# Where the second network's rounding runs, when the first network's last sums leave their banks, and when the last weights are split

## The reference

```python
h = np.maximum(x @ w_in, 0.0)            # first network, 1536 tokens, 512 -> 2048
x = h * h @ w_out                        # 2048 -> 512

h = x @ w_in2                            # second network, same sizes
P = a[0] + a[1] * h + a[2] * h**2 + a[3] * h**3
Q = 1.0 + np.abs(b[0]) * np.abs(h) + np.abs(b[1]) * h**2
out = (P / (Q + 1e-06)) @ w_out2
```

## Time and profile before

| | |
|---|---|
| median of 3 runs | 607.12 us (606.97 to 607.15) |
| profiled execution, device time | 609.34 us |
| profiled execution, span from first to last instruction | 607.6 us |
| PE, PEld | 590.7 us (97%), 481.3 us (79%) |
| DVE, ACT, POOL | 444.5 us (73%), 263.7 us (43%), 153.6 us (25%) |
| mean granted TensorE clock | 0.994 |

### The profile page before, as it was taken

One profiled execution on the slowest core, in us unless ns is written; L12 is line 12 of the kernel. 1 busy time (PEld: TensorE's weight loads), 2 busy tenths in 40 slices (PEclk: granted clock), 3 DMA queues, 4 the chain that ended last, 5 costly groups with the idle time before them and its releaser, 6 DMA issues.

```text
span 607.6 us, 10584 instructions
## 1 busy us (share of the span) xinstructions
PE 590.7 (97%) x3770; PEld 481.3 (79%) x3770; DVE 444.5 (73%) x834; ACT 263.7 (43%) x564; POOL 153.6 (25%) x163
## 2 busy tenths in 40 slices
PE   7988999999999999999999899999999999999996
PEld 4877788888888888888888677788888888888884
DVE  5878796664433323466674799999999999999996
ACT  4988611011310111301112855556766665766554
POOL 3679810000300000400000755521222212222220
PEclk9999999999999999999999999999999999999998
DMA  8883470000000000022232000000100000100001
GB/s 260 256 236 116 150 277 0 1 0 1 1 0 0 0 0 0 35 81 93 105 105 104 35 1 0 1 0 1 69 0 0 0 0 0 71 0 1 0 1 69
DMA packets 11186, 31.42 MB, mean 52 GB/s; under 512 B 1552, under 2 KB 2064, under 8 KB 11152
## 3 DMA queue, kind: packets, MB, share of 16 engines
q1 hardware_dynamic: 10864, 30.68, 15.3%
q10 hardware_dynamic: 288, 0.26, 0.1%
HBM read 27.79 MB, written 3.15 MB: 51 GB/s over the span
## 4 chain that ended last, share of the span: by engine, by line
PE 49%; DVE 35%; issue 8%; ACT 4%; POOL 3%; DVEq 1%; POOLq 0%
PE bank L520 22%; PE bank L587 21%; DVE ratio L982 9%; DVE numer L964 6%; DVE ratio L976 5%; DVE numer L962 5%; DVE ratio L971 5%; DVE hhi L989 4%; ACT prob L668 2%; POOL prob L354 1%; PE bank L602 1%; PE bank L506 1%; PE bank L490 1%; POOL vwin L339 1%; PE bank L545 1%
## 5 line engine op out<-in xcount | busy, mean ns | idle before, releaser
L520 PE MATMUL bank<-xhi,whi 128*128 (+1 forms) x384 | 149.9, 390 | 0.0
L520 PE MATMUL bank<-xhi,wlo 128*128 (+1 forms) x384 | 149.4, 389 | 0.0
L520 PE MATMUL bank<-xlo,whi 128*128 (+1 forms) x384 | 149.4, 389 | 0.0
L407 POOL TENSOR_TENSOR denom<-denom,habs 128x512 f32<-128x512 f32 (+1 forms) x49 | 62.2, 1271 | 252.5 <-ACT denom L746 252.5
L685 ACT ACTIVATE hsq<-bank 128x512 f32<-128x512 f32 x48 | 28.8, 600 | 213.2 <-PE bank L520 213.1
L520 PEld LDWEIGHTS bank<-xhi,wlo 128*128 128x128 f32 x384 | 72.2, 188 | 15.2
L520 PEld LDWEIGHTS bank<-xhi,whi 128*128 128x128 f32 x384 | 72.2, 188 | 15.0
L520 PEld LDWEIGHTS bank<-xlo,whi 128*128 128x128 f32 x384 | 72.0, 188 | 14.7
L602 PE MATMUL bank<-whi,hhi 128*128 128x512 f32 x192 | 76.8, 400 | 6.2 <-DVE hlo L993 6.2
L602 PE MATMUL bank<-wlo,hhi 128*128 128x512 f32 x192 | 76.2, 397 | 0.0
L602 PE MATMUL bank<-whi,hlo 128*128 128x512 f32 x192 | 75.9, 396 | 0.0
(11 more groups left out here) (76 smaller groups left out, 896.3 us busy)
## 6 DMA issues: line engine op xcount, KB each, us to landing
wraw<-w SPq DMA_DIRECT2D x32, 512.0 KB, 3.3
vwin<-vw SPq DMA_DIRECT2D x16, 288.0 KB, 5.2
out<-osb SPq DMA_DIRECT2D x12, 256.0 KB, 2.1
kraw<-kT SPq DMA_DIRECT2D x7, 384.0 KB, 5.3
q<-qT SPq DMA_DIRECT2D x7, 384.0 KB, 4.1
kraw<-kT SPq DMA_DIRECT2D x2, 128.0 KB, 2.3
q<-qT SPq DMA_DIRECT2D x1, 256.0 KB, 4.9
kraw<-kT ACTq DMA_DIRECT2D x1, 128.0 KB, 2.8
```

The lines of the kernel that those rows point to most:

```text
L407: g.tensor_tensor(denom[:, i, cols], denom[:, i, cols], habs[:, i, cols], ALU.mult).then_inc(q_done, 1)
L520: last = mm(hps[j % 2][:, :], W[a][:, j, kt * P:(kt + 1) * P], X[b][:, kt, bass.ds(CH * c, CH)], start=kt == 0 and i == 0, stop=kt == KT - ...
```

## The change

1. The rounding of `ratio` to `hhi` (`high`) moves from VectorE to ScalarE. On ScalarE the rounding of tile m-1 stands inside `terms` of tile m, behind its `denom` and ahead of its `numer`. For the last tile, which is done in two halves, the roundings stand behind both exponentials. VectorE's order for the two halves of the last tile is changed with it.
2. The four banks of the first network's last sums are emptied by four plain copies (`y_raw`) that stand behind tile 1's reciprocal, where eight copies stood between tile 1's `terms` and its reciprocal. Each bank's rounded copy (`y_hi`) is made later from `xraw`, one behind each of the tiles 2 to 5. GpSimd takes the four differences behind the tiles 13, 15, 17 and 19. The row copies of a finished chunk (`rows_out`) also move behind tile 1's reciprocal.
3. `LATE` is 3 and not 4, so VectorE splits the weights of tile 12. GpSimd splits the six halves of the tiles 13 to 15 behind the tiles 0, 3, 5, 7, 9 and 11, the halves for `hidden` first, where it split eight halves behind the tiles 2 to 9. The sums of the tiles 13 to 15 wait for their own half (`late_out`).

The core of the diff:

```diff
-LATE = 4
+LATE = 3
...
-        product(0, 0)
-        product(1, 1)
-        y_lo(NCH - 1)
-
-        for x in range(2 * LATE):
-            product(2 + x, x % 2)
-            j = FT - LATE + x // 2
+        def split_late(j, half):
             index, turn = landing(FT + j)
             pool.wait_ge(w_in[index], 16 * (turn + 1))
-            split(half_slot(j, x % 2), w_hi_pool, 2 * EARLY + x, w_late)
...
+        product(0, 0)
+        split_late(FT - 3, 0)
+        product(1, 1)
+        between = [None, lambda: split_late(FT - 2, 0), lambda: split_late(FT - 1, 0)]
+        between += [lambda j=j: split_late(j, 1) for j in range(FT - LATE, FT)]
+        between += [lambda dt=dt: y_lo_last(dt) for dt in range(KT)]
+        for pair in range(1, len(between)):
+            product(2 * pair, 0)
+            product(2 * pair + 1, 1)
+            between[pair]()
...
+            if j >= FT - LATE:
+                pe.wait_ge(late_out, j - FT + LATE + 1)
...
-                        pe.wait_ge(ylo_done, KT * NCH)
+                        pe.wait_ge(ylo_done, KT * c + 2 * KT)
...
+        def y_raw(dt):
+            bank_done(y_done, NCH - 1, dt, KT, STEPS - 1)
+            a.copy(xraw[last_y(dt)], acc[dt][:, :].unsqueeze(1)).then_inc(y_free, 1)
+
+        def y_hi(dt):
+            act.wait_ge(y_free, done(KT, KT * (NCH - 1) + dt))
+            a.copy(xhi[last_y(dt)], xraw[last_y(dt)]).then_inc(yhi_done, 1)
...
+        def high(m, i, cols=WHOLE, tile=None):
+
+            act.wait_ge(ratio_done, m + 1)
+            act.wait_ge(b_done, done(2, STEPS + (m if tile is None else tile) - 2))
+            a.copy(hhi[:, i, cols], ratio[:, cols]).then_inc(hi_done, 1)
...
-            for cols in parts:
+            for part, cols in enumerate(parts):
                 a.activation(denom[:, i, cols], habs[:, i, cols], ACT.Identity, bias=cb[:, 0:1],
                              scale=cb[:, 1:2]).then_inc(den_done, 1)
+                if part == 0 and not first:
+                    high(m - 1, 1 - i)
...
+        rational(0, 0, first=True)
+        rational(1, 1)
+        for dt in range(KT):
+            y_raw(dt)
+        for dt in range(KT):
+            rational(2 + dt, dt % 2)
+            y_hi(dt)
...
+        for half, cols in enumerate(HALVES):
+            high(LAST + half, 1, cols, LAST)
         rows_out(NCH - 1)
...
-            for step in (newton_1, newton_2, product, high, low):
+            for step in (newton_1, newton_2, product, low):
                 step(m, i, i)
...
         newton_1(*first)
         newton_2(*first)
+        product(*first, LAST)
         newton_1(*second)
-        product(*first, LAST)
         newton_2(*second)
-        high(*first, LAST)
+        low(*first)
         product(*second, LAST)
-        low(*first)
-        high(*second, LAST)
         low(*second)
```

More of the change, by code:

```diff
@@ L212, in build @@
     w_in_ready, w_out_hi, w_out_ready = sem("w_in_ready"), sem("w_out_hi"), sem("w_out_ready")
-    w_late = sem("w_late")
+    late_in, late_out = sem("late_in"), sem("late_out")
     h_full = sem("h_full")
@@ L393, in _, with y_lo @@
             split_out(j)
-        def y_lo(c):
+        def y_lo(c, dt):
+            part = (slice(None), dt, slice(CH * c, CH * (c + 1)))
+            g.tensor_tensor(xlo[part], xraw[part], xhi[part].bitcast(F32), ALU.subtract).then_inc(ylo_done, 1)
+        for c in range(NCH - 1):
             for dt in range(KT):
                 pool.wait_ge(y_free, done(KT, KT * c + dt))
[L398 to L402, removed]
+                y_lo(c, dt)
         def product(m, i, cols=WHOLE):
@@ L407, in product, with y_lo_last @@
             g.tensor_tensor(denom[:, i, cols], denom[:, i, cols], habs[:, i, cols], ALU.mult).then_inc(q_done, 1)
-        product(0, 0)
-        product(1, 1)
-        y_lo(NCH - 1)
-        for x in range(2 * LATE):
-            product(2 + x, x % 2)
-            j = FT - LATE + x // 2
+        def split_late(j, half):
             index, turn = landing(FT + j)
             pool.wait_ge(w_in[index], 16 * (turn + 1))
-            split(half_slot(j, x % 2), w_hi_pool, 2 * EARLY + x, w_late)
-        with pool.Fori(2 + 2 * LATE, STEPS - 2, 2) as m:
+            split(half_slot(j, half), w_hi_pool, 2 * EARLY + LATE * half + j - FT + LATE, (late_in, late_out)[half])
+        def y_lo_last(dt):
+            pool.wait_ge(yhi_done, KT * (NCH - 1) + dt + 1)
+            y_lo(NCH - 1, dt)
+        product(0, 0)
[8 more added lines that the diff above has]
+            between[pair]()
+        with pool.Fori(2 * len(between), STEPS - 2, 2) as m:
             for i in range(2):
@@ L528, in weights_ready @@
             elif index >= 2 * FT - LATE:
-                pe.wait_ge(w_late, 2 * (index - 2 * FT + LATE + 1))
+                pe.wait_ge(late_in, index - 2 * FT + LATE + 1)
             else:
@@ L723, in y_out, with last_y @@
                 a.copy(xraw[part], acc[dt][:, :].unsqueeze(1)).then_inc(y_free, 1)
+        def last_y(dt):
+            return slice(None), slice(dt, dt + 1), slice(CH * (NCH - 1), TOK)
+        def y_raw(dt):
[4 more added lines that the diff above has]
+            a.copy(xhi[last_y(dt)], xraw[last_y(dt)]).then_inc(yhi_done, 1)
         relu(1, 1)
@@ L735, in _, with terms @@
                     relu(FT * c + j + i, i)
-        def terms(m, i, parts=(WHOLE,)):
+        def high(m, i, cols=WHOLE, tile=None):
+            act.wait_ge(ratio_done, m + 1)
+            act.wait_ge(b_done, done(2, STEPS + (m if tile is None else tile) - 2))
+            a.copy(hhi[:, i, cols], ratio[:, cols]).then_inc(hi_done, 1)
+        def terms(m, i, parts=(WHOLE,), first=False):
             n = STEPS + m
@@ L756, in reciprocal, with rational @@
             a.activation(rcp0[bank][:, cols], rcp0[bank][:, cols], ACT.Exp, scale=-1.0).then_inc(r0_done, 1)
[L758 to L761, removed]
+        def rational(m, i, first=False):
+            terms(m, i, first=first)
             reciprocal(m, i, i)
@@ L770, in _, with tiles, chunk @@
         act.wait_ge(coef_step, 3)
[L771 to L774, removed]
+        def tiles(c, first, last):
+            with act.Fori(first, last, 2) as j:
                 for i in range(2):
                     rational(FT * c + j + i, i)
-        chunk(0, lambda: y_out(NCH - 1))
+        def chunk(c, last=FT):
+            rational(FT * c, 0)
+            rational(FT * c + 1, 1)
+            rows_out(c - 1)
+            tiles(c, 2, last)
+        rational(0, 0, first=True)
[5 more added lines that the diff above has]
+            y_hi(dt)
+        tiles(0, 2 + KT, FT)
         with act.Fori(1, NCH - 1) as c:
-            chunk(c, lambda: rows_out(c - 1))
-        chunk(NCH - 1, lambda: rows_out(NCH - 2), final=True)
+            chunk(c)
+        chunk(NCH - 1, FT - 2)
         rational(LAST - 1, 0)
@@ L983, in product @@
                                    ALU.subtract, ALU.mult).then_inc(ratio_done, 1)
[L985 to L989, removed]
         def low(m, i, bank, cols=WHOLE):
```

## The result

The changed kernel takes 599.73 us in the median of 6 executions (598.44 to 602.83), the kernel before on the same chips 608.12 us (6 executions, 606.97 to 610.51). The ratio is 0.9872, with a 95% interval of 0.9849 to 0.9895: 1.3% faster, some 7.8 us; the two medians lie 8.39 apart. The prediction had 598.7 us and a range of 597.2 to 602.0.

The account below looks back on a forecast made before the run. It took TensorE, busy 97% of the span, plus its waits for `hlo` as the bound. Gains of 8.12 us at the change of networks and 0.3 at the end, 8.4, off 607.12 gave 598.7 us, range 597.2 to 602.

Parts of the forecast that it names:

- The change of networks: From the second network's sums 0 to sums 9: waiting 2.28, slow clock 1.74, slow tiles 4.10, all recovered, 8.12 us.
- The layout of one tile: Steady tile, from its `habs` start: `hlo` done at 8.8 us, sums want it at 10.7, 1.9 us to spare.
- The margins of the race: `ratio` starts ahead of GpSimd's next product by 0.7 us in steady tiles, 0.2 at tiles 2, 18 and 34.
- the 4.10 us of the slow stretch: Seven steps, sums 2 to 9, where VectorE and GpSimd block each other: 4.10 us lost, put at fully recovered.
- The end: Last two sums: gaps of 0.5 and 1.7 us, last matmul 1.4 us earlier, less 1.1 for clock, gain 0.3.
- the clock: Gap ahead of sums 47 may halve TensorE's clock, costing 2.2 us; half of it, 1.1, taken off the gain.
- the sum: 8.12 us at the change of networks plus 0.3 at the end: 8.4 us off 607.12, giving 598.7.
- Rival 1: GpSimd's product starts before `ratio`: 5.9 us a tile; 611.1 us from tile 18, 618 from tile 2; chance 0.10.
- Rival 2: `ratio` starts late from tile 2, won back by tile 8 or so: costs about 4 us, 602.8 us; chance 0.06.

Follow-up runs that it names:

- e4: The changed kernel with the weight halves as before (LATE 4, eight halves behind tiles 2 to 9): 601.94 us, ratio 0.9897.
- e8: The changed kernel with the rounding to `hhi` back on VectorE: 606.25 us, ratio 0.9966.
- e3: The kernel before with only the weight halves moved (LATE 3, VectorE splits tile 12): 606.11 us, ratio 0.9970.
- e2: The kernel before with only the bank and row copies and GpSimd's four differences moved, rounding on VectorE: 607.25 us, ratio 0.9992.
- e12: The changed kernel with bank copies, row copies and GpSimd's four differences where they were before: 626.11 us, ratio 1.0267.
- e1: The kernel before with only the rounding to `hhi` moved to ScalarE: 626.79 us, ratio 1.0268.
- e6: The changed kernel with an unused 256-column copy added on ScalarE behind the row copies of chunks 1 and 2: 614.86 us, ratio 1.0117.
- e9: The changed kernel run again, unchanged, in six more executions: 599.61 us, ratio 0.9841.
- e11: The changed kernel with each group's fourth copy behind `denom` of the chunk's tile 2, plus an unused 256-column ScalarE copy: 601.58 us, ratio 0.9889.
- e5: The changed kernel plus an unused 64-column ScalarE copy behind chunks 1 and 2's row copies: 598.64, 599.12, 612.95 and 614.36 us; ratio 0.9846 for the short two.
- e10: The changed kernel with each group's fourth copy behind tile 2's `denom`, and tile 46's rounding behind both halves of tile 47's `denom`: 601.16 us, ratio 0.9878.

## Why the prediction was right

**The change of networks, 8.12 us.** All of it came back: the steps 0 to 11 lose nothing. The layout of one tile held: in tile 10 `hlo` is done 8.80 us behind that tile's `habs`, where the prediction has 8.8, and the sums start at 10.60, where it has 10.7. The rounding takes 0.62 us where 0.66 was put in, as the group of ACT shows; with it the groups of DVE and POOL, 320 to 600 us (busy us, mean ns, idle before):

```profile
L1029 DVE TENSOR_TENSOR hlo<-ratio,hhi 128x512 fp32r<-128x512 f32 x47 | 50.1, 1065 | 34.6 <-ACT hhi L764 34.6
L1024 DVE SCALAR_TENSOR_TENSOR ratio<-numer,ca,ratio 128x512 f32<-128x512 f32 x47 | 35.3, 752 | 5.7
L764 ACT CAST hhi<-ratio 128x512 fp32r<-128x512 f32 x47 | 29.1, 620 | 13.1 <-DVE ratio L1024 12.2
L407 POOL TENSOR_TENSOR denom<-denom,habs 128x512 f32<-128x512 f32 x47 | 64.3, 1368 | 241.5 <-ACT denom L775 241.5
```

`ratio` takes 0.75 us in every tile; in a steady tile before it was 1.28. `hlo` is lengthened instead, to 1.07 in the mean, where TensorE has slack, and VectorE idles 34.6 us for the rounding at no cost. (The Trainium skill, VectorE: DVE Perf Modes, the cycle table under the TRN2 errata, gives an estimate of 0.61 us for this rounding; the trace agrees, 0.62.)

The margins of the race were forecast as 0.2 at tile 2, 0.2 at tiles 18 and 34 and 0.7 in between. The trace has 0.11, 0.19 and 0.20, and 0.71 in the steady stretch. After each of the three the margin comes back by 0.1 a tile. The timeline of DVE and POOL after, at tile 2:

```profile
345.86 0.75 DVE L1024 SCALAR_TENSOR_TENSOR ratio<-numer,ca,ratio 128x512 f32<-128x512 f32 x1
...
345.97 1.79 POOL L407 TENSOR_TENSOR denom<-denom,habs 128x512 f32<-128x512 f32 x1 [3.55 <-ACT denom L775]
```

**What it did not see.** The prediction took the 4.10 us of the slow stretch as recovered by all parts together, with the rarer weight halves named as one reason. The runs put it down to the rounding: without the halves' new places it is all recovered (e4), without the rounding only 0.3 of it is (e8, 3.8 lost). The halves alone gave 2.6 us (e3, of which 2.2 in the first two steps). And the four differences on GpSimd, which the prediction passed over, would cost 1.9 us in the steps 12 to 19 if VectorE still rounded (e2, e8). What the rounding hides is thus 3.8 + 1.9 + 0.2 at these places and 1.4 at the end (there together with VectorE's new order for the last tile, which e8 also takes back): 7.3 of the 9.49. The copies and the splits give the other 2.2, and the copies keep the race from being lost at tile 1 (e12).

**The end.** The gaps were to be 0.5 and 1.7 us. Counted as the prediction counts them, by how much later the sums start than they could, they are 0.49 and 1.78; the idle times in the rows are 0.33 and 1.53. The last matmul was to start 10.1 behind the last tile's `habs`, and it starts 10.12 behind it (583.81 to 593.93). The loss at the end is 2.4 instead of 3.8, the 1.4 of the prediction. The term that was off is the clock: the prediction took off 1.1, half of what a lower clock would cost in the last sums, and the profiled execution shows none, nor does any other with a gap of 1.48 to 1.53 us at this place (e1, e4, e6, e9, e11). This is the difference between the 9.49 measured and the 8.4 of the sum. That the median lies 1.0 above the forecast all the same is not explained by a step of it: the kernel before has a median of 608.12 over six executions and of 607.12 over the three from which the forecast subtracted. So it is luck in part that the two medians lie 8.39 apart and the sum has 8.4: the sum contains a clock cost of 1.1 that no trace of this kernel shows.

The end also shows that the low clock before was not what made it late. In e8 (and e2) the gap ahead of sums 46 is as long, the clock stays at 1.00, and the end loses the same 3.8 us, because a second gap opens ahead of sums 47. The slow matmuls before had only covered that wait. What came back is the shorter way to the last `hlo`. PE in e8, and the window behind the first gap:

```profile
593.45 0.47 PE L613 MATMUL bank<-whi,hhi 128*128 128x512 f32 x1 [1.95 <-DVE hlo L1031]
...
597.73 0.47 PE L613 MATMUL bank<-whi,hhi 128*128 128x512 f32 x1 [1.31 <-DVE hlo L1031]
...
593.40:597.70 4.30, 2.97 (x12) 2.17 (x12) 4.23 (x11) 0.00 (x0) 0.00 (x0) 1.00 0.00 0
```

**Rival 1** is real, and its price was right. It was worked out as 5.9 us a tile and is 5.80 to 5.87, with `ratio` at 1.46 us and not near 1.2. From tile 18 it was to cost 12.4 us; the e5 execution that lost there loses 15.7 from sums 0 on against 2.4, so 13.3, and took 612.95 against the 611.1 of the prediction. The prediction let a start be decided by 0.1 us and gave this case 0.10. In 12 executions of the changed kernel it did not come true: the highest is 602.83, and where the race was lost at tile 18 the time was above 612. Lost at tile 34 it would cost, as an estimate from the same rows, 12 tiles of 0.4 us and the 1.8 by which the end of e5 is dearer, some 6.6.

**Rival 2**, a loss won back, was not seen in a trace. Once lost, the margin does not grow back: in e12 it is -0.38 us in nearly every tile from 12 to 45. In e5 it was won once, at tile 33, where the row copies push GpSimd's next product 2.0 us back (tile 34's `habs` comes 7.86 us behind tile 33's, where 5.8 is usual in this state), and lost again in the next tile.

**What stays open.** Of the 12 executions of the changed kernel (e9's with it) three lie at 601.89 to 602.83 us, with a mean granted clock of 0.997 or 0.994; the nine at 598.4 to 600.9 have 1.000. None of the three was profiled. A race lost for good it is not, since that costs 6.6 us at the least. The profiled execution of e4 (601.29 us, mean clock 0.997) shows one place where such time can lie: from sums 0 on it loses 2.3 us like the changed kernel, but far ahead of the networks, in the attention, its clock is lowered. The windows from 30 to 45 us, of e4 and then of the changed kernel:

```profile
30.00:45.00 15.00, 13.04 (x302) 10.38 (x296) 10.50 (x59) 10.95 (x49) 9.19 (x13) 0.89 0.69 216
...
30.00:45.00 15.00, 13.77 (x368) 11.06 (x360) 12.26 (x71) 13.14 (x59) 11.17 (x16) 1.00 0.83 241
```

The profiled execution of e6, the longest of its four, has 0.77 from 15 to 30 us and 0.89 from 30 to 45, and its sums 0 start at 345.18. Nor does a wide margin make the scatter smaller (e10: 600.09 to 603.72, e11: 600.67 to 605.17). The short loss at tile 2 that rival 2 describes is thus not needed to explain these executions, but no run rules it out. Whether the 0.11 us at tile 2 is always enough is open too: 0.08 was in two traces, 0.05 was not in one.

## What to carry to other kernels

Where two engines share a resource that the first one holds for its whole instruction, don't ask only how long each is busy. Lay out the two starts for the worst tile of a period, write down the margin, and work out the loop that closes if the second one comes first: if its length is above the bound's step, one lost start costs all steps that follow. Test the margin by adding a few hundred nanoseconds of idle work ahead of it. And judge the parts of such a change together, since the part that brings most of the gain here (7.3 of 9.49 us) makes the kernel, alone, 2.7% slower.

## What was unexpected

The same program has two times 14 us apart, 598.6 to 599.1 and 613.0 to 614.4, when the two starts lie within 0.04 us by the trace (e5). Which of them comes is decided anew in each execution.

Whoever comes second still has most of its own work ahead when the other is done. GpSimd's product, started 0.11 us behind `ratio`, ends 1.15 us behind its end (347.76 against 346.61; undisturbed it takes 1.29), and `ratio`, started behind a product, 0.55 behind the product's end (undisturbed 0.75). So it pays a little less than the other's rest: 0.50 us where `ratio` had 0.64 left, and in e1 0.71 where the product had 0.91 left. (The Trainium skill, SBUF — State Buffer, section on the two separate sides, gives the rule, that the first one to start holds the port pair for its whole instruction; the trace agrees, but these times behind the end are from the traces alone.)

The length of a gap alone does not tell whether TensorE's clock is lowered behind it. Gaps of 1.86 and 2.12 us lowered it before, and so did one of 1.96 in e3 and 2.03 in e5 and in e12. But it stayed at 1.00 behind gaps of 1.95 in e8, 1.85 in e2, 2.06 in e6 and 2.01 and 2.57 in e1. Behind the gaps up to 1.78 us that these traces have in the second network it was never lowered, 1.53 in the changed kernel among them.
